# Attention and two expert layers on one core: all inputs laid out on the host, q and pooled k, v arrive with the head dimension on the partitions

## The reference

```python
k_p = k.reshape(B, H, Sp, pool, D).mean(axis=3)      # pool = 8, Sp = 72
v_p = v.reshape(B, H, Sp, pool, D).mean(axis=3)
scores = scale * np.matmul(q, k_p.transpose(0, 1, 3, 2))
attn = softmax(scores)
x = (attn @ v_p) as (B*S, H*D) = (4608, 512)
# soft mixture of experts: 32 slots, 8 experts of 4 slots
logits = x @ phi
d = softmax(logits, over tokens);  slot_input = d.T @ x
h = np.maximum(slot_input[e] @ w1[e], 0.0);  slot_out[e] = h @ w2[e]
c = softmax(logits, over slots);   x = c @ slot_out
# second layer
h = x @ w_in;  solu = h * softmax(h)
out = (layernorm(solu) * g_ln) @ w_out
```

## Time and profile before

| what | us |
|---|---|
| median of 3 runs | 451.15 (450.9 to 452.35) |
| span of the profiled execution, first to last instruction | 449.2 |
| TensorE (PE) busy | 431.4 (96%) |
| VectorE (DVE) busy | 316.9 (71%) |
| ScalarE (ACT) busy | 267.4 (60%) |
| GpSimd (POOL) busy | 251.0 (56%) |

### The profile page before, as it was taken

How to read it: one execution, slowest core, us unless ns; L and a number is a source line. 1 busy time by engine, 2 the same in 40 slices (tenths; PEclk the granted TensorE clock), 3 DMA queues, 4 the chain that set the end, 5 groups by cost and what they waited for, 6 DMA issues and landing times.

```text
span 449.2 us, 10103 instructions
## 1 busy us (share of the span) xinstructions
PE 431.4 (96%) x3492; PEld 335.0 (75%) x3492; DVE 316.9 (71%) x558; ACT 267.4 (60%) x604; POOL 251.0 (56%) x347
## 2 busy tenths in 40 slices
PE   6899999999999998999899999999999999999997
PEld 6676787778778775445578788888888888888886
DVE  5888697877879665736598987777777777777311
ACT  2588878778787854134387665655565555666310
POOL 2569977878887230112034336766766667666540
PEclk9999999999999999999999999999999999999999
DMA  8969959898999998999500276676666766666642
GB/s 258 296 190 239 257 151 267 329 283 279 341 211 359 388 393 285 392 389 396 207 1 24 48 163 118 132 144 137 134 136 140 141 134 134 132 118 136 154 81 47
DMA packets 125951, 91.71 MB, mean 204 GB/s; under 512 B 105176, under 2 KB 105440, under 8 KB 124000
## 3 DMA queue, kind: packets, MB, share of 16 engines
q1 hardware_dynamic: 120752, 82.08, 66.8%
q10 hardware_dynamic: 5168, 9.24, 6.0%
HBM read 66.13 MB, written 9.44 MB: 168 GB/s over the span
## 4 chain that ended last, share of the span: by engine, by line
PE 75%; DVE 7%; ACT 6%; DMA 6%; issue 3%; POOL 1%; SPq 1%; DVEq 0%; ACTq 0%
PE banks L1835 13%; PE banks L1837 13%; PE banks L1836 13%; PE banks L1412 5%; DMA wslot<-in_moe_w 5%; PE banks L1475 3%; PE banks L1393 3%; PE banks L1807 3%; ACT vpad L685 2%; PE banks L1499 2%; PE banks L1535 2%; PE banks L1698 2%; PE banks L1506 2%; PE banks L1720 2%; DVE attn L1039 1%
## 5 line engine op out<-in xcount | busy, mean ns | idle before, releaser
L1835 PE MATMUL banks<-wo_hi,uh 128*128 128x512 f32 x280 | 109.6, 391 | 0.1
L1837 PE MATMUL banks<-wo_hi,ul 128*128 128x512 f32 x280 | 109.0, 389 | 0.0
L1836 PE MATMUL banks<-wo_lo,uh 128*128 128x512 f32 x280 | 108.9, 389 | 0.0
L653 POOL TENSOR_TENSOR ul<-u_col,uh 128x1024 fp32r<-128x1024 f32 x30 | 72.2, 2407 | 16.2 <-ACT uh L685 15.0
L577 POOL TENSOR_TENSOR attn<-attn,srec 128x576 f32<-128x576 f32 (+1 forms) x40 | 43.2, 1082 | 39.6 <-DVE srec L1051 39.4
L950 ACT ACTIVATE sq<-u,st 128x1024 f32<-128x1024 f32 x36 | 41.5, 1153 | 39.9 <-DVE u L1284 39.9
L1835 PEld LDWEIGHTS banks<-wo_hi,uh 128*128 128x128 f32 x280 | 52.6, 188 | 11.4 <-DVE ul L1301 0.5
L1837 PEld LDWEIGHTS banks<-wo_hi,ul 128*128 128x128 f32 x280 | 52.5, 188 | 11.0
L1836 PEld LDWEIGHTS banks<-wo_lo,uh 128*128 128x128 f32 x280 | 52.6, 188 | 10.7
L1284 DVE SCALAR_TENSOR_TENSOR u<-banks,ex 128x1024 f32<-128x1024 f32 x35 | 42.7, 1223 | 22.3 <-ACT ex L941 22.2
L1274 DVE TENSOR_REDUCE st<-banks 128x1 f32<-128x1024 f32 x35 | 42.6, 1218 | 17.5 <-PE banks L1807 17.5
(11 more groups left out here) (197 smaller groups left out, 792.8 us busy)
## 6 DMA issues: line engine op xcount, KB each, us to landing
wslot<-in_moe_w SPq DMA_DIRECT2D x13, 2048.0 KB, 13.6
u_col<-u_blk SPq DMA_DIRECT2D x240, 64.0 KB, 2.2
qb<-in_q SPq DMA_DIRECT2D x32, 256.0 KB, 6.3
out<-osb ACTq DMA_DIRECT2D x32, 256.0 KB, 2.5
vraw<-in_v SPq DMA_DIRECT2D x8, 640.0 KB, 5.4
kraw<-in_k SPq DMA_DIRECT2D x7, 640.0 KB, 5.9
vraw<-in_v SPq DMA_DIRECT2D x8, 512.0 KB, 4.0
kraw<-in_k SPq DMA_DIRECT2D x7, 512.0 KB, 5.0
```

Source lines behind the costliest of these rows:

```text
L653: pool.tensor_tensor(ul[par][:, :, :].rearrange("p c (q t) -> p (c q) t", q=4), v, uh[par][:, :, :].bitcast(F32).rearrange("p c (q t) -> p ...
L1835: pe.matmul(ps[4 + par], uh[par][:, c, :], wo_hi[:, c, :], start=(c == 0), stop=False)
L1836: pe.matmul(ps[4 + par], uh[par][:, c, :], wo_lo[:, c, :], start=False, stop=False)
L1837: last = pe.matmul(ps[4 + par], ul[par][:, c, :], wo_hi[:, c, :], start=False, stop=(c == FC - 1))
```

## The change

- **q**: the host gives it as 128 rows for each batch, with the two heads of a pair times 64 dimensions on the partitions, tile by tile. It is one transfer for each batch (two for batch 0), 9216 bytes for each partition. `qT_t`, `qT_evac`, and the tile `qT` are gone; `scores` reads `qb` directly.
- **k, v**: the same layout, the 8 rows to be averaged in separate stretches of 72 columns. The folds are over 1152, 576 and 288 elements. The result has the head dimension on the partitions, so `kT_t`, `vT_t` and their evictions are gone; `kblk_fill` and `vpad_fill` are two ScalarE copies each from SBUF, 64 partitions by 288. v folds right into `vT` (now two buffers), and `vT_copy`, `vT_close` are gone.
- **v72**: `v72_t` of batch b+1 moves from step 2 of the batch itself to step 5 of the batch before, ahead of `vphi_t`, into a bank of its own. `v72_evac` moves from step 3 to step 1, `vpad_fill` from step 4 to step 3.
- **weights**: w1, w2, w_in, w_out come in runs of a partition's whole share (16 KB for a half of w1 or w2). The loads of the expert weights start a batch earlier (`b >= 2`). The load of `wslot3`'s second place waits for the last `vphi_ps` now.
- **g_ln** arrives transposed, so its transpose and copy are gone.
- Tiles are placed elsewhere in SBUF.

```diff
@@ sync: loads
-            def load_q(b, par, tiles=range(TILES)):
-                for t in tiles:
-                    if t < 4:
-                        sp.dma_start(qb[par][:, t, :].rearrange("p (h d) -> p h d", h=H), row(q_main[:, t], b)).then_inc(sem(f"q_in{par}{t}"), 16)
...
+            def load_q(b, par):
+                sp.dma_start(qb[par][:, :], row(q, b)).then_inc(sem(f"q_in{par}"), 16)
...
             load_first_k()
-            load_q(0, 0, (0, 1))
+            load_first_q(0, 2, "q_first")
             load_v(0)
-            load_q(0, 0, (2, 3))
+            load_first_q(2, TILES, "q_in0")
...
-                sp.wait_ge(sem("qT_ps"), b * TILES)
+                sp.wait_ge(sem("s_ps"), b * TILES)
                 load_q(b + 1, 1 - b % 2)
-                if b >= 3:
-                    load_w((b - 3) // 2, (b - 3) % 2)
-                if b == 6:
-                    load_w(2, 0)
+                if b >= 2:
+                    load_w((b - 2) // 2, (b - 2) % 2)
...
@@ scalar
-            def kT_evac(b, par, hh):
...
+            def kblk_fill(b, par, hh):
+
+                act.wait_ge(sem("k_pooled"), b + 1)
+                copy(kblk_half(par, hh), kp[hh * D:(hh + 1) * D, :, :], 1.0 / POOL / D ** 0.5).then_inc(sem("kT_half" if hh == 0 else "kT_sb"), 1)
+
+            def vpad_fill(b, par):
+                act.wait_ge(sem("v_pooled"), b + 1)
                 for hh in range(2):
-                    one_half("vT", b, lambda hh: vpad[hh * D:(hh + 1) * D, :, 1 + hh * HEAD:1 + hh * HEAD + SP], 1.0 / POOL, hh)
...
+                    last = copy(vpad_half(hh), vT[par][hh * D:(hh + 1) * D, :, :], 1.0 / POOL)
+                last.then_inc(sem("vT_sb"), 1)
...
-                if t == 3:
+                if t == 3 and first:
+                    v72_evac(b, par)
+                if t == 1 and not first:
                     v72_evac(b, par)
                 if t == (2 if first else 1) and not last:
-                    kT_evac(b + 1, 1 - par, 0)
+                    kblk_fill(b + 1, 1 - par, 0)
                 if t == 2 and not last:
-                    kT_evac(b + 1, 1 - par, 1)
-                if t == 4 and not last and not first:
-                    vT_evac(b + 1)
+                    kblk_fill(b + 1, 1 - par, 1)
+                if t == 3 and not last and not first:
+                    vpad_fill(b + 1, 1 - par)
...
@@ vector
-                if t == 4 and not first and not last:
-                    vT_copy(b + 1)
...
@@ tensor
             def scores(tile, early=False):
                 b, par, t = tile
-                g = num(tile)
-                pe.wait_ge(sem("qT_sb"), g + 1)
+                if not early:
+                    pe.wait_ge(sem("s_sub"), num(ahead(b, par, t - 1)) + 1)
...
-                        last = pe.matmul(s_view[:, j, 0:2 * SP], qT[bit(tile)][:, j, :], kblk[par][:, j, :], start=True, stop=True)
+                        last = pe.matmul(s_view[:, j, 0:2 * SP], q_cols(par, t, j), kblk[par][:, j, :], start=True, stop=True)
...
-                if t == 2:
-                    v72_t(b)
+                if t == 2 and first:
+                    v72_t(b, par)
...
                 if t == 5:
+                    v72_t(b + 1, 1 - par)
                     vphi_t(b + 1)
```

More of the change, by code:

```diff
@@ L56 @@
 WARM = 26
-SPLIT = 3
+QCOLS = PAIRS * S
 AHEAD = 5
@@ L134, in build @@
         attn_end = place[0]
[L135 to L142, removed]
         kblk.append(bump("kblk1", [P, PAIRS, 2 * SP]))
-        qT = [bump(f"qT{i}", [P, PAIRS, P]) for i in range(2)]
+        vT = [bump(f"vT{i}", [P, PAIRS, SP]) for i in range(2)]
+        assert place[0] >= attn_end + HALF // MC
         aT = [bump(f"aT{i}", [P, NB, P]) for i in range(2)]
-        early_end = place[0]
+        vphi = [bump(f"vphi{i}", [P, NB, SLOTS]) for i in range(2)]
+        assert place[0] <= attn_end + HALF
+        place[0] = attn_end + HALF
+        tail = place[0]
         v72 = [bump(f"v72_{i}", [SP, H, D]) for i in range(2)]
+        cs = [at(f"cs{i}", [P, TILES, 4, SLOTS], F32, tail + i * size([P, TILES, 4, SLOTS])) for i in range(2)]
+        place[0] = tail + 2 * size([P, TILES, 4, SLOTS])
         smax = [bump(f"smax{i}", [P, H]) for i in range(2)]
@@ L378, in out_steps, with fold, part @@
                 step(i, i, 0)
-        def fold(engine, name, raw, pooled, b, level):
-            w = 4 * D >> level
+        def fold(engine, name, raw, pooled, b, level, used=None):
+            def part(first, n):
+                return raw[:, :, first:first + n, :].rearrange("p j i m -> p j (i m)")
+            n = 4 >> level
             if level == 0:
[L385 to L393, removed]
-                engine.tensor_tensor(pooled[:, :, :], raw[:, :, 0:w], raw[:, :, w:2 * w], ALU.add).then_inc(sem(f"{name}_pooled"), 1)
+                engine.wait_ge(sem(f"{name}_in"), b * 16 + 16)
+            else:
+                engine.wait_ge(sem(f"{name}_fold"), b * 2 + level)
+            if level < 2:
+                engine.tensor_tensor(part(0, n), part(0, n), part(n, n), ALU.add).then_inc(sem(f"{name}_fold"), 1)
+                return
+            if used is not None:
+                engine.wait_ge(sem(used[0]), used[1])
+            engine.tensor_tensor(pooled[:, :, :], raw[:, :, 0, :], raw[:, :, 1, :], ALU.add).then_inc(sem(f"{name}_pooled"), 1)
         block = ctx.enter_context(nc.Block())
@@ L799, in step @@
                     datT_evac(b - 1)
-                if not (last and t + 3 >= TILES):
-                    qT_evac(ahead(b, par, t + 3))
                 if t == 5:
@@ L1585, in step @@
                     keep_clock(b_tail, 3)
-                if not (last and t + 3 >= TILES):
-                    qT_t(ahead(b, par, t + 3))
                 if t == 4 and not first:
                     dat_t(b - 1, 1 - par, (4,))
-                if t == 2 and first:
-                    kT_t(b + 1)
                 if t == 1 and first:
@@ L1597, in step @@
                     scores(ahead(b, par, t + 2))
-                if t == 4 and first:
-                    vT_t(b + 1)
                 if not first:
@@ L1606, in step @@
                         slot_t(b - 1, 1 - par)
-                if t == 1 and not first and not last:
-                    kT_t(b + 1)
                 if t == 1 and first:
@@ L1628, in step @@
                         datT_t(b - 1)
-                if t == 3 and not last and not first:
-                    vT_t(b + 1)
                 if t == 4 and not last and not first:
```

336 lines of the change are left out of this document (117 added, 219 removed).

## The result

The changed kernel takes 440.5 us (median of 4 runs, 439.66 to 441.92), the kernel before 451.02 in the same session: a ratio of 0.9748, 95% interval 0.972 to 0.9777. The profiled execution has a span of 438.9 us for 449.2.

| stretch | before | forecast | after |
|---|---|---|---|
| start, to vphi of batch 1 | 40.38 | 37.3 | 38.38 |
| six batches of the loop | 117.83 | 108.2 | 107.23 |
| vphi of batch 7 to hid(0) | 20.40 | 20.2 | 20.37 |
| hid(0) to the eighth expert's output | 37.59 | 36.6 | 36.54 |
| from there to the first output matmul | 12.42 | 12.4 | 12.88 |

A forecast was written before the change was run, and what follows sets the result against it. It took TensorE as the loop's bound, then a chain ending mostly on VectorE. Loop 9.6, start 3.1, loop end 0.2 and experts 1.0 sum to 13.9 off 449.2: 435.3, plus 1.95 for the median, 437.2; range 428.5 to 444.3.

The forecast's parts named there:

- TensorE's share: In the loop, dropped transposes of q, pooled v and k save TensorE 3.1 us a batch; about half is given back.
- The walk through the five subtractions: In the loop, VectorE's subtraction ends, followed tile by tile, give 18.05 us a batch, 9.6 saved over six.
- Rivals 2: In the loop, TensorE stays the bound: 16.5 us a batch, 428.2 in all; chance 0.12.
- 3 (19.3): In the loop, fixed-order waits take nearly all back: 19.3 us a batch, 444.8 in all; chance 0.18.
- Tile 6 to 7: In a loop batch, from one subtraction's end to the next: 3.62 us falls to 3.25 without the vT copies.
- vpad_fill ahead of the eviction: In the loop, tile 5 to 6: two vpad copies on ScalarE ahead of the logits' eviction, charged at 0.35 us.
- Start, 3.1: In batch 0, earlier pooled k, faster vpad pieces and shorter folds save 3.1 us; first maximum near 9.8.
- The clock: In the loop, more TensorE idling might halve its clock and double 16.5 us a batch; left inside a 0.04 chance.
- End of stretch 1, 0.2: In the last batch of the loop, only g's transpose and copy go: 0.2 us saved.
- Stretch 2, 1.0: In the experts' matmuls after the loop, faster weight loads remove TensorE's 1.01 us wait: 1.0 saved, nothing beyond.
- rival 4: In the experts' weight loads after the loop, long rows load badly: slower, 461 us; chance 0.04.
- Stretch 3 is matmuls that the change doesn't touch: From the first output matmul to the end, nothing changes: 220.55 us before and after.

The follow-up runs named there:

- b2: The changed kernel with 18 transposes per batch put back on TensorE in the loop, nobody waiting for them: 445.88 us.
- d1: The changed kernel with two 64x288 copies per batch put back on VectorE where the vT copies stood, nobody waiting for them: 440.61 us.
- c1: The changed kernel with 320 unused bytes ahead of wo0, 38 transposes for 26 ahead of the first scores, and vpad_fill behind dat_evac: 437.46 us.
- a3: The changed kernel with 32 more unused bytes behind gT, so that wslot starts 64 bytes behind its old place: 440.82 us.
- a1: The changed kernel with the 32 bytes of gT moved back, so that wslot stands at its address of before: 440.86 us.
- b4: The changed kernel with vpad_fill behind the two aT copies of its step: 441.69 us.
- c3: The changed kernel with the experts' weights left in the old layout and loaded in the old short runs: 442.13 us.
- b1: The changed kernel with 320 unused bytes ahead of wo0, so that wo_lo stands 35840 bytes behind wo_hi: 438.35 us.
- c2: The kernel before with 192 unused bytes ahead of wo0, so that wo_lo stands 35520 bytes behind wo_hi: 454.12 us.
- a2: The kernel before with 32 unused bytes ahead of wslot and nothing else: 451.74 us.
- b3: The changed kernel with one copy per tile put back on ScalarE where the q copies stood, nobody waiting for it: 446.99 us.
- a4: The changed kernel with 60 transposes in place of 26 ahead of the first scores: 441.47 us.

## Why the prediction held, step by step

- **The size, 437.2 against 440.5**, within the range and short by 3.3 us: 2.95 in stretch 3, 1.1 at the start, 0.5 behind stretch 2 and 0.2 at the end of stretch 1, less 1.0 that the loop gave more, 0.05 in stretch 2, and 0.35 because the median lies 1.6 us above the span and not 1.95. That the loop's surplus covered a third of stretch 3's loss was luck.
- **TensorE's share, 3.1 us a batch, half of it given back.** Right in its result: 1.77 came of 3.1. The walk through the five subtractions gave 18.05 and 17.87 was measured, cycle by cycle within 0.2. Rivals 2 (16.5 a batch) and 3 (19.3) are out by 1.4 us on either side. The words "VectorE's chain ends last in four of five places" were too strong: b2 shows that 2.0 us more of TensorE cost 0.89, so TensorE and ScalarE are links of the same ring.
- **Tile 6 to 7, the vT copies' place, 3.25.** Measured 3.19, and d1 shows that the copies themselves had become free there.
- **vpad_fill ahead of the eviction, charged at 0.35.** About right: 0.28 a batch came back in c1.
- **Start, 3.1.** 2.0 came. The path was right (a3 has its first maximum at 9.81), the term "1.22 of matmuls" failed: at the lower clock they took 2.26. I had weighed the clock against the loop alone and not against the gap that the earlier transposes leave in front of the first scores.
- **The clock.** The Trainium skill (TensorE: Matmul & The Clock Gate, Why this matters for your kernels) warns that long idle gaps between bursts of matmuls bring TensorE to half its clock. The fall behind the gap of 2.30 us at the start goes the way of that warning. The loop has only gaps of under 1 us, so the doubling that I had worked out for it does not follow from the page, and it did not come: three traces (a1, a3, b4) show one fall in the loop, at 1.0 to 1.1 us each. Why the clock falls there is not shown.
- **End of stretch 1, 0.2.** 0.03 came, nothing that can be told from none.
- **Stretch 2, 1.0.** 1.05 came, and c3 shows the cause. The rate went up to 424 to 426 GB/s from 387 to 420, so rival 4 fell. The Trainium skill (DMA: Bandwidth & Descriptors, Latency and other measured facts) advises, for copies of 16 KB a partition between HBM tensors whose rows lie far apart, to pad the rows or to lay the tiles out contiguously; loads are not what it measured there, and no run here shows such a copy. "Nothing beyond this 1.0 can be had" missed what came next: the chain behind the last expert, hidden under the wait before, cost 0.46.
- **"Stretch 3 is matmuls that the change doesn't touch".** This step failed, by 2.95 us. It touched where they read: wo_lo lies 192 bytes elsewhere (b1, c2).

## What to carry to other kernels

A change of layout also moves what is not in the diff of a stage: print the addresses of the operands of the longest loop before and after, and if a loop without gaps runs 1.6% slower with unchanged instructions, move one operand by a few hundred bytes before looking for anything else. In a ring of waits no engine alone is the bound: put one engine's share back and measure. When work ahead of a chain gets shorter, look at what then stands still: here the first scores behind a gap of 2.30 us ran at the lower clock and took 2.26 us for 1.22.

## What the runs showed of the hardware

- Placing wo_lo, one of the operands that TensorE streams (128x512), 192 bytes elsewhere made matmuls of 128x512 follow each other at 226 to 236 ns for 226 or 227, in all four lines of the loop, those that don't read it too; a shift of all operands by 32 or 64 bytes together (32: a2 against the kernel before, a3 against the changed kernel; 64: a3 against a1) changed nothing.
- TensorE's clock stayed at 1.00 behind 26 transposes and a gap of 1.18 to 1.62 us (a3, b3, b4, c3) and fell to 0.50 behind 26 transposes and a gap of 1.88 to 2.44 us (the changed kernel, a1, b1, b2, d1). It also fell behind shorter gaps: in the loop (a1, a3, b4) at 1.0 to 1.1 us each and at the end of stretch 1 (a2, c1) at 1.7, with gaps of at most 0.65 us in the 10 us before, and in batch 0 (c3) at 1.9, with gaps of up to 1.23.
- Transposes alone brought TensorE from its lower level to its higher one: after 17 to 26 of them the distance from start to start went from 213 to 109 ns, while the row of the granted clock read 1.00 throughout (before, the changed kernel, a4, c1).
- Loads of 16 KB a partition, contiguous in HBM, ran at 424 to 426 GB/s with TensorE fully busy, runs of 2 and 4 KB at 391 and 397.
